# Loading q and k of an attention kernel already transposed, spreading them by transfers, and ranking clusters in PSUM

## Chip, cores and metric

One core of a Trainium2 chip runs the whole program. The metric is the device time of one execution in microseconds; the median of three runs of the kernel before is 873.62 us (873.53 to 875.32).

## What is computed

Three layers, one after the other, all in float32. The attention has 16 heads (2 batches of 8), 768 tokens and a head dimension of 64. Every query and every key is assigned to the nearest of 16 centroids of its head, and a query sees only keys of its own cluster:

```python
q_assign = argmax(einsum('bhsd,hcd->bhsc', q_n, c_n))   # k_assign alike
mask = q_assign[:, :, :, None] == k_assign[:, :, None, :]
scores = where(mask, q @ k^T / 8, -1e9)
attn = softmax(scores);  x = attn @ v          # -> [1536 tokens, 512]
h = x @ w_in;  g = P(h) / Q(|h|);  y = g @ w_out            # 512 -> 2048 -> 512
out = (silu(y @ w_gate) * (y @ w_val)) @ w_out2             # 512 -> 1536 -> 512
```

## The kernel before

Every float32 factor of a matmul is split into a high part, rounded to the fast matmul type, and a low part, the rest; products of the parts are added in PSUM. The five engines each run their own list of instructions, written out by hand and tied by semaphores. The attention is a software pipeline over `STEPS`: step i brings the scores of tile i (128 queries of a head against its 768 keys), six steps to a head, and the later stages of older tiles follow with fixed lags. The two layers behind it (`mlps`, `mlp1`, `hidden`, `first_result`, `second_result`) come after the last step, except for four units of the first one that run in the last steps.

In one step TensorE (PE) issues the four score matmuls of its tile (L854, L857), six transposes of the probabilities of tile i-5 (L877) and a third of the product with v (L892, L894). VectorE (DVE) takes the row maximum (L699), and the low parts of the transposed probabilities (L719, two halves); every third step it adds an epsilon to three row sums (L708) and inverts them (L711), and once in three steps it forms x (L728). ScalarE (ACT) takes the exponential of the tile before (L513), the high parts of the transposed probabilities (L534) and half of x (L544). GpSimd (POOL) scales three tiles by their inverses every third step (L404), splits x (L412, L414), v (L422, L425), and the first six units of the weights of the first layer (L432, L434; one in each of the steps 23, 35, 47, 59, 90 and 93).

`head_at(step, stage)` names the head whose preparation has this stage at this step: stage s of head h falls at step 6h-13+s. In the kernel before they are:

- stage -1: POOL splits q and k, 128 tokens in the partitions (L391, L394), into `qk_split`
- stages 1 to 3: PE transposes four blocks of it each (L915), ACT copies them from PSUM to `qkT` (L558, L561), whose upper partitions so hold the high parts and whose lower ones hold the low parts
- stages 4 and 5: PE multiplies with the centroids (L933); ACT copies the low products (L576), DVE adds them (L734) and takes the maximum (L738)
- stage 6: DVE marks the maximum (L742), weighs by rank (L748) and takes the first (L752)
- stage 7: DVE makes the one-hot codes (L689); stage 8: PE transposes them (L866), ACT copies them to `clusterT` (L522, L524)

SyncE (SP) issues every DMA, in one queue. Its loop over heads waits for `qkT` of head h and for the scores of head h-2, issues four copies of 192 KB into `k_hihi` and `qk_low` (L294), waits for `clusterT` of head h, issues six copies of it (L297), and then the loads of q and k of head h+2 (L256), of v (L263) and, for the first four heads, of weights (L268, L271). The scores of head h wait for all ten copies (`s_dup`). Weight units 4 and up are loaded behind the attention's buffers that they replace.

Of the kernel before, what the change touches and what calls it, by code (L numbers as in the profile page):

```python
# [21 lines left out]
def build_program(nc, q, k, v, centroids, w_in, w_out1, a, b, w_gate, w_val, w_out2, out):  # L22
    P = 128
    B, H, S, D = q.shape
# [127 lines left out]
    HID, RES = 0, 4  # L152

# [13 lines left out]
    s_qkhi, s_qklo = sem("s_qkhi"), sem("s_qklo")  # L167
    s_tr, s_trc = sem("s_tr"), sem("s_trc")
# [24 lines left out]
    FIRST_STEP = -PREP_LEAD - 1  # L193
# [8 lines left out]
    def prep_bank(h, stage):  # L202

        return stage - 1 if h == 0 else PREP

# [40 lines left out]
    with block:  # L246

        @block.sync
        def _(sp):
            def load_qk(h):  # L250
                i, src = h % 2, (h // H, h % H)
                if h >= 2:

                    sp.wait_ge(s_qklo, h - 1)
                for n, t in enumerate((q, k)):
                    sp.dma_start(qk_raw[i][:, n, :, :],  # L256
                                 t[src[0], src[1]].rearrange("(p t) d -> p t d", t=T)
                                 ).then_inc(s_qk_in[i], 16)
# [21 lines left out]
            sp.dma_start(b_raw, b[None, :].to_broadcast([P, 2])).then_inc(s_par_in, 16)  # L280
            for h in range(NH):
                i = h % 2

                sp.wait_ge(s_trc, 3 * (h + 1))
# [4 lines left out]
                kT = qkT[h % 3][:, T:2 * T, :].rearrange("p t n -> p (t n)")  # L289
                qT = qkT[h % 3][:, 0:T, :].rearrange("p t n -> p (t n)")  # L290
# [16 lines left out]
            for u in range(EARLY, NF1):  # L307
                if w1_end(u) <= PREP_END:

                    sp.wait_ge(s_tr, 3 * NH)  # L310
                    sp.wait_ge(s_ohT, NH)
                    sp.wait_ge(s_dup[(NH - 1) % 2], DUPS * ((NH + 1) // 2))
                elif w1_end(u) <= PROB_END:
                    sp.wait_ge(s_pT, 2 * NT)
                else:
                    sp.wait_ge(s_xlo, NG)
# [12 lines left out]
            rows = out.rearrange("(c p t) d -> c t p d", c=B, t=T)  # L329
            for bl in range(NB):  # L330
                for tt in range(TT):
# [3 lines left out]
                    sp.dma_start(rows[tile // T, tile % T],  # L335
# [4 lines left out]
        def _(pool):  # L340
# [43 lines left out]
            for step in STEPS:  # L384
                h = head_at(step, -1)
                if h is not None:

                    pool.wait_ge(s_qk_in[h % 2], 32 * (h // 2 + 1))
                    if h:
                        pool.wait_ge(s_tr, 3 * h)  # L390
                    did(g.tensor_scalar(qk_split[:, :, :, 0, :].bitcast(F32R), qk_raw[h % 2][:, :, :, :],  # L391
                                        1.0, 1.0, ALU.mult, ALU.mult), s_qkhi)
                    pool.wait_ge(s_qkhi, h + 1)
                    did(g.tensor_tensor(qk_split[:, :, :, 1, :].bitcast(F32R), qk_raw[h % 2][:, :, :, :],  # L394
                                        qk_split[:, :, :, 0, :], ALU.subtract), s_qklo)
                    if h < 2:
                        g.memset(qk_low[h][0:D, :, :].bitcast(F32), 0.0).then_inc(s_zero, 1)

                if (step - HALF) % HALF == 0 and 0 <= (step - HALF) // HALF < NG:
                    half = (step - HALF) // HALF  # L400
                    pool.wait_ge(s_inv, half + 1)
                    for n in range(HALF):
                        i = (half * HALF + n) % T
                        did(g.tensor_scalar(prob[i][:, :], prob[i][:, :], row_inv[:, i:i + 1], 1.0,  # L404
                                        ALU.mult, ALU.mult), s_norm)
                g1, third = pv_at(step)
                if third == HALF - 1:

                    pool.wait_ge(s_xsum, g1 + 1)
                    finish_last()  # L410
                    xh, xl, raw = x_of(x_hi, g1), x_of(x_lo, g1), x_of(x_raw, g1)
                    did(g.tensor_scalar(xh, raw, 1.0, 1.0, ALU.mult, ALU.mult), s_xhi)  # L412
                    pool.wait_ge(s_xhi, g1 + 1)
# [28 lines left out]
        def _(sc):  # L442
# [62 lines left out]
            for step in STEPS:  # L505
# [10 lines left out]
                h = head_at(step, 8)  # L516
# [29 lines left out]
                for stage in (1, 2, 3):  # L546
                    h = head_at(step, stage)
                    if h is None:
                        continue

                    sc.wait_ge(s_tr, 3 * h + stage)
                    if h >= 3 and stage == 1:
                        sc.wait_ge(s_score, T * (h - 2))
                    n = 4 * (stage - 1)
                    nq = min(max(T - n, 0), 4)
                    src = ps[:, prep_bank(h, stage), :].rearrange("p (k n) -> p k n", k=4)
                    if nq:
                        ins = s.activation(qkT[h % 3][:, n:n + nq, :], src[:, 0:nq, :], ACT.Copy,  # L558
                                           scale=QSCALE)
                    if nq < 4:  # L560
                        ins = s.activation(qkT[h % 3][:, n + nq:n + 4, :], src[:, nq:4, :], ACT.Copy)  # L561
                    ins.then_inc(s_trc, 1)
                if head_at(step, 3) == 0:
# [6 lines left out]
                h = head_at(step, 5)  # L570
# [14 lines left out]
        def _(ve):  # L585
# [97 lines left out]
            for step in STEPS:  # L683
                h = head_at(step, 7)
                if h is not None:
                    if h:
                        ve.wait_ge(s_ohT, h)
                    ve.wait_ge(s_first, h + 1)
                    v_.tensor_tensor(onehot[:, :, :], ranked[:, :, :],  # L689
# [11 lines left out]
                if (step - HALF) % HALF == 0 and 0 <= (step - HALF) // HALF < NG:  # L701
# [29 lines left out]
                h = head_at(step, 5)  # L731
                if h is not None:
                    ve.wait_ge(s_logit_lo, h + 1)
                    v_.tensor_tensor(logit[:, :, :], ps[:, PREP, 0:4 * T * C].rearrange(  # L734
                        "p (n two c) -> p n two c", two=2, c=C)[:, :, 0, :], logit_lo[:, :, :],
                        ALU.add).then_inc(s_logit_sum, 1)
                    ve.wait_ge(s_logit_sum, h + 1)
                    v_.tensor_reduce(top[:, :], logit[:, :, :], AX.X, ALU.max).then_inc(s_top, 1)  # L738
                h = head_at(step, 6)
                if h is not None:  # L740
                    ve.wait_ge(s_top, h + 1)
                    v_.tensor_tensor(is_top[:, :, :], logit[:, :, :],  # L742
                                     top[:, :].unsqueeze(2).to_broadcast([P, 2 * T, C]),
                                     ALU.is_equal).then_inc(s_istop, 1)
# [3 lines left out]
                    v_.tensor_tensor(ranked[:, :, :], is_top[:, :, :],  # L748
                                     ramp[:, :].unsqueeze(1).to_broadcast([P, 2 * T, C]), ALU.mult
                                     ).then_inc(s_ranked, 1)  # L750
                    ve.wait_ge(s_ranked, h + 1)
# [227 lines left out]
```

## Time and profile before

| what | value |
|---|---|
| median of three runs | 873.62 us |
| the profiled execution | 873.85 us |
| its span, first to last instruction | 872.1 us |
| busy over the span: PE, DVE, ACT, POOL | 825.4, 545.5, 446.5, 383.5 us |
| mean granted TensorE clock | 0.996 of full speed |
| DMA: packets, bytes | 44012, 45.39 MB |

The busy time of an engine is the union of its instructions; PE's matmuls overlap, and their ends are modelled. "L404" is line 404 of the kernel before. In the rows below, what stands in brackets or behind the bar is the idle time of the engine ahead of an instruction and who ended it.

### The profile page before, as it was taken

What the parts mean: (1) busy time and instruction counts of PE and PEld (TensorE: products, weight loads), DVE (VectorE), ACT (ScalarE), POOL (GpSimd) and SP (SyncE); (2) the same over time, 40 slices, a digit from 0 to 9 for tenths busy, and PEclk for the clock granted to TensorE, in tenths of its full rate; (3) what the DMA queues carried; (4) which work ended last, traced back from release to release, by engine and by line L of the source; (5) the groups of instructions that cost most, each with busy time, mean ns of one, the idle gap of its engine ahead of it and who ended that gap; (6) DMA issues with size and microseconds to landing.
All of it is one profiled execution on the core that took longest, in us unless ns stands there. A gap on an engine that the chain in (4) does not pass through costs nothing.

```text
span 872.1 us, 11981 instructions
## 1 busy us (share of the span) xinstructions
PE 825.4 (95%) x4210; PEld 705.2 (81%) x4210; DVE 545.5 (63%) x911; ACT 446.5 (51%) x876; POOL 383.5 (44%) x352
## 2 busy tenths in 40 slices
PE   4789898898999989999999999999999999999998
PEld 3688887888888778888888888878888888888886
DVE  4698998988999868777877787753221321231222
ACT  3488777787788778777877787720000100010001
POOL 4467877878676849851222156696000000000000
PEclk9999999999999999999999999999999999999999
DMA  3634242232423034000000023340000100010001
GB/s 96 159 99 114 78 105 69 75 95 68 106 71 82 30 101 141 0 1 1 1 1 0 1 73 110 108 145 1 1 0 1 49 1 0 1 49 1 0 1 49
DMA packets 44012, 45.39 MB, mean 52 GB/s; under 512 B 5040, under 2 KB 34736, under 8 KB 43952
## 3 DMA queue, kind: packets, MB, share of 16 engines
q1 hardware_dynamic: 43952, 44.62, 18.2%
q8 instruction: 34, 0.56, 0.3%
q14 instruction: 26, 0.21, 0.1%
HBM read 27.30 MB, written 3.15 MB: 35 GB/s over the span
## 4 chain that ended last, share of the span: by engine, by line
PE 78%; DVE 14%; POOL 3%; issue 2%; ACT 1%; DMA 0%; SPq 0%; DVEq 0%; POOLq 0%; ACTq 0%
PE ps L766 17%; PE ps L765 17%; PE ps L767 17%; DVE neg_max L699 4%; PE ps L877 4%; PE ps L837 4%; PE ps L838 4%; PE ps L839 4%; DVE probT_lo L719 3%; PE ps L892 2%; PE ps L894 2%; PE ps L933 2%; PE ps L854 2%; PE ps L915 2%; PE ps L857 2%
## 5 line engine op out<-in xcount | busy, mean ns | idle before, releaser
L765 PE MATMUL ps<-x_hi,w_hi 128*128 128x512 f32 x480 | 186.8, 389 | 0.0
L766 PE MATMUL ps<-x_lo,w_hi 128*128 128x512 f32 x480 | 186.8, 389 | 0.0
L767 PE MATMUL ps<-x_hi,w_lo 128*128 128x512 f32 x480 | 186.7, 389 | 0.0
L671 DVE TENSOR_TENSOR act<-act,ps 128x512 f32<-128x512 f32 x36 | 24.8, 688 | 209.9 <-PE ps L767 209.9
L502 ACT ACTIVATE act<-ps 128x512 f32<-128x512 f32 x36 | 21.5, 598 | 249.5 <-PE ps L767 249.5
L366 POOL TENSOR_TENSOR den<-den,mag 128x512 f32<-128x512 f32 x48 | 62.3, 1299 | 122.5 <-ACT den L463 122.2
L404 POOL TENSOR_SCALAR prob<-prob,row_inv 128x768 f32<-128x768 f32 x96 | 85.8, 911 | 49.7 <-DVE row_inv L711 49.6
L877 PE MATMUL ps<-ident,prob 128*128 128x128 f32 x576 | 82.5, 279 | 24.4 <-DVE probT_lo L719 22.6
L767 PEld LDWEIGHTS ps<-x_hi,w_lo 128*128 128x128 f32 x480 | 90.1, 188 | 18.8
L765 PEld LDWEIGHTS ps<-x_hi,w_hi 128*128 128x128 f32 x480 | 90.1, 188 | 18.7
L766 PEld LDWEIGHTS ps<-x_lo,w_hi 128*128 128x128 f32 x480 | 90.1, 188 | 18.5
L719 DVE TENSOR_TENSOR probT_lo<-ps,probT_hi 128x384 fp32r<-128x384 f32 x192 | 97.3, 548 | 11.5 <-ACT probT_hi L534 11.3
L699 DVE TENSOR_REDUCE neg_max<-ps 128x1 f32<-128x768 f32 x96 | 91.4, 952 | 16.2 <-PE ps L857 14.8
L534 ACT ACTIVATE probT_hi<-ps 128x384 fp32r<-128x384 f32 x192 | 84.5, 493 | 25.1 <-PE ps L877 23.2
L877 PEld LDWEIGHTS ps<-ident,prob 128*128 128x128 f32 x576 | 65.9, 141 | 38.0 <-issue 29.1
L513 ACT ACTIVATE prob<-ps,neg_max 128x768 f32<-128x768 f32 x96 | 86.9, 905 | 15.2 <-DVE neg_max L699 14.7
L765 PE MATMUL ps<-g_hi,w_hi 128*128 128x512 f32 x192 | 74.7, 389 | 0.0
L766 PE MATMUL ps<-g_lo,w_hi 128*128 128x512 f32 x192 | 74.7, 389 | 0.0
L767 PE MATMUL ps<-g_hi,w_lo 128*128 128x512 f32 x192 | 74.7, 389 | 0.0
L892 PE MATMUL ps<-probT_hi,v_split 128*128 128x384 f32 x192 | 73.2, 381 | 1.3 <-DVE x_raw L728 1.3
L894 PE MATMUL ps<-probT_lo,v_split 128*128 128x384 f32 x192 | 65.2, 339 | 0.0
L854 PE MATMUL ps<-k_hihi,qkT 128*128 128x384 f32 x192 | 57.4, 381 | 0.2
(98 smaller groups left out, 1555.6 us busy)
## 6 DMA issues: line engine op xcount, KB each, us to landing
w_raw<-in_moe_w_out SPq DMA_DIRECT2D x28, 256.0 KB, 4.2
k_hihi<-qkT SPq DMA_DIRECT2D x32, 192.0 KB, 3.0
qk_low<-qkT SPq DMA_DIRECT2D x32, 192.0 KB, 3.7
w_raw<-in_moe_w_in SPq DMA_DIRECT2D x16, 256.0 KB, 3.9
qk_raw<-in_q SPq DMA_DIRECT2D x16, 192.0 KB, 2.7
qk_raw<-in_k SPq DMA_DIRECT2D x16, 192.0 KB, 2.6
v_raw<-in_v SPq DMA_DIRECT2D x16, 192.0 KB, 3.2
w_raw<-in_moe_w_gate SPq DMA_DIRECT2D x12, 256.0 KB, 3.1
```

The source lines that it names most:

```text
L404: did(g.tensor_scalar(prob[i][:, :], prob[i][:, :], row_inv[:, i:i + 1], 1.0, ALU.mult, ALU.mult), s_norm)
L513: s.activation(prob[i % T][:, :].rearrange("p (c n) -> p c n", c=2), ps[:, bank:bank + 2, 0:HC], ACT.Exp, bias=neg_max[:, i % T:i % T + 1] ...
L534: s.activation(probT_hi[g % 2][:, n * HALF:(n + 1) * HALF, c:c + P], ps[:, PT_BANK + n, 0:HC].rearrange("p (k n) -> p k n", k=HALF), ACT.C ...
L699: v_.tensor_reduce(neg_max[:, i % T:i % T + 1], ps[:, bank:bank + 2, 0:HC], AX.XY, ALU.max, negate=True).then_inc(s_max, 1)
L719: v_.tensor_tensor(probT_lo[g % 2][:, keys, c:c + P], ps[:, PT_BANK + n, 0:HC].rearrange("p (k n) -> p k n", k=HALF), probT_hi[g % 2][:, k ...
L765: mm(dst, hi, m_hi, start=start, stop=False)
L766: mm(dst, hi, m_lo, start=False, stop=False)
L767: return mm(dst, lo, m_hi, start=False, stop=stop)
L854: mm(ps[:, bank + c, 0:HC], qkT[h % 3][:, t, :], k_hihi[sl][:, c * HC:(c + 1) * HC], start=True, stop=False)
L877: last = transpose(ps[:, PT_BANK + n, kt % HALF * P:(kt % HALF + 1) * P], prob[i % T][:, kt * P:(kt + 1) * P], ident[:, :])
L892: mm(ps[:, O_BANK, 0:HC], vv, probT_hi[g % 2][:, kt, :], start=(kt == 0), stop=False)
L894: last = mm(ps[:, O_BANK, 0:HC], vv, probT_lo[g % 2][:, kt, :], start=False, stop=(kt == T - 1))
```

## The change

q arrives in DRAM as [head, 64, 768], and k likewise with its tokens in the order that the transposed tiles had (the host lays them out before the launch, so no device time is in that). One load puts q into the upper 64 partitions of `qk_raw` and k into the lower ones. POOL scales q by 1/8 in place, ACT rounds both to `qk_hi`, POOL subtracts for `qk_lo`, and SP spreads the parts by four transfers of 192 KB per head into `qkT`. The 12 transposes and four ACT copies per head are gone. The sums and codes of the ranking stay in the PSUM bank that held the products, and the ranking is cut at other steps; the last copy of the codes comes one step later. The epsilon of the row sums moves from DVE to POOL. x is split once for two heads, 128 partitions at a time. `PREP_END` shrinks, so `POOL_UNITS` is 5 in place of 6: weight unit 5 is loaded and split behind the attention. q's tokens keep their natural order, so the rows of the output do, too. Stages in the changed kernel: scale and high part 0, low part 2, products 4 and 5, sum 6, rank 7, first and one-hot 8, cluster 9.

```diff
     place = region(W_AT + EARLY * 8 * U1, T_AT)
-    qk_raw = [place(f"qk_raw{i}", [P, 2, T, D]) for i in range(2)]
-    qk_split = place("qk_split", [P, 2, T, 2, D])
+    raw_at = [cursor[0] + i * 4 * S for i in range(2)]
+    qk_raw = [place(f"qk_raw{i}", [P, S]) for i in range(2)]
+    qk_lo = [at(f"qk_lo{i}", [P, S], F32R, raw_at[i]) for i in range(2)]
+    qk_hi = [place(f"qk_hi{i}", [P, S], F32R) for i in range(2)]
     logit_lo = place("logit_lo", [P, 2 * T, C])
-    logit = place("logit", [P, 2 * T, C])
-    is_top = place("is_top", [P, 2 * T, C])
-    ranked = place("ranked", [P, 2 * T, C])
...
+    pair = ps[:, PREP, 0:4 * T * C].rearrange("p (n two c) -> p n two c", two=2, c=C)
+    logit, is_top = pair[:, :, 0, :], pair[:, :, 1, :]
...
+    S_SCALE, S_HI, S_LO, S_CEN, S_LOGIT, S_SUM, S_RANK, S_FIRST, S_CLUSTER = 0, 0, 2, 3, 4, 6, 7, 8, 9
+    def qkT_ready(h):
+        return s_qkT_in[h % 3], 64 * (h // 3 + 1)
+    def x_pair(x, h):
+        col = (h // H) * S
+        return x[:, (h % H) // 2, col:col + S]
...
@@ SP @@
+                    sp.wait_ge(*qkT_ready(h - 2))
+                    sp.dma_start(qk_raw[i][n * D:(n + 1) * D, :], t[src[0], src[1]]
+            def spread_qk(h):
+                i, dst = h % 2, qkT[h % 3].rearrange("p t n -> p (t n)")
+                if h >= 3:
+                    sp.wait_ge(s_score, T * (h - 2))
+                sp.wait_ge(s_qkhi, h + 1)
+                for n in range(2):
+                    sp.dma_start(dst[0:D, n * S:(n + 1) * S].bitcast(F32),
+                                 qk_hi[i][n * D:(n + 1) * D, :].bitcast(F32)
+                                 ).then_inc(s_qkT_in[h % 3], 16)
+                sp.wait_ge(s_qklo, h + 1)
+                for n in range(2):
+                    sp.dma_start(dst[D:P, n * S:(n + 1) * S].bitcast(F32),
+                                 qk_lo[i][n * D:(n + 1) * D, :].bitcast(F32)
+                                 ).then_inc(s_qkT_in[h % 3], 16)
+            spread_qk(0)
             for h in range(NH):
-                sp.wait_ge(s_trc, 3 * (h + 1))
+                sp.wait_ge(*qkT_ready(h))
...
                     sp.dma_start(dst.bitcast(F32), src.bitcast(F32)).then_inc(s_dup[i], 16)
+                if h + 1 < NH:
+                    spread_qk(h + 1)
                 sp.wait_ge(s_cluster, 2 * (h + 1))
@@ POOL, ahead of the steps @@
+            for i in range(2):
+                g.memset(qk_low[i][0:D, :, :].bitcast(F32), 0.0).then_inc(s_zero, 1)
@@ POOL, in a step: scale of q; epsilon and scaling of prob; low part; x; v; weights @@
+                h = head_at(step, S_SCALE)
+                    pool.wait_ge(s_qk_in[h % 2], 32 * (h // 2 + 1))
+                    did(g.tensor_scalar(qk_raw[h % 2][0:D, :], qk_raw[h % 2][0:D, :], QSCALE, 1.0,
+                                        ALU.mult, ALU.mult), s_qscale)
...
+                    pool.wait_ge(s_exp, HALF * (half + 1))
+                    did(g.tensor_scalar(row_den[:, c:c + HALF], row_sum[:, c:c + HALF], EPS_SUM, 1.0,
+                                        ALU.add, ALU.mult), s_den)
                     pool.wait_ge(s_inv, half + 1)
...
+                h = head_at(step, S_LO)
+                    pool.wait_ge(s_qkhi, h + 1)
+                    did(g.tensor_tensor(qk_lo[h % 2][:, :], qk_raw[h % 2][:, :],
+                                        qk_hi[h % 2][:, :].bitcast(F32), ALU.subtract), s_qklo)
-                if third == HALF - 1:
+                if third == HALF - 1 and g1 % 4 == 3:
...
-                    xh, xl, raw = x_of(x_hi, g1), x_of(x_lo, g1), x_of(x_raw, g1)
+                    xh, xl, raw = x_pair(x_hi, h), x_pair(x_lo, h), x_pair(x_raw, h)
@@ ACT, in a step behind exp, cluster copies, high parts of prob and x_part; logit_lo (S_SUM) follows @@
+                h = head_at(step, S_HI)
+                    sc.wait_ge(s_qscale, h + 1)
+                    if h >= 2:
+                        sc.wait_ge(*qkT_ready(h - 2))
+                    s.activation(qk_hi[h % 2][:, :], qk_raw[h % 2][:, :], ACT.Copy).then_inc(s_qkhi, 1)
...
@@ DVE @@
-                    ve.wait_ge(s_exp, HALF * (half + 1))
-                    v_.tensor_scalar(row_den[:, c:c + HALF], row_sum[:, c:c + HALF], EPS_SUM, None,
-                                     ALU.add).then_inc(s_den, 1)
                     ve.wait_ge(s_den, half + 1)
+                    v_.tensor_tensor(logit, logit, logit_lo[:, :, :], ALU.add).then_inc(s_logit_sum, 1)
+                    v_.tensor_tensor(is_top, logit, top[:, :].unsqueeze(2).to_broadcast([P, 2 * T, C]),
+                    v_.tensor_tensor(is_top, is_top, ramp[:, :].unsqueeze(1).to_broadcast([P, 2 * T, C]),
@@ PE: stages 1 to 3 are gone; ahead of the products with the centroids @@
-                    pe.wait_ge(s_trc, 3 * h + 3)
+                    pe.wait_ge(*qkT_ready(h))
+                    if h:
+                        pe.wait_ge(s_cluster, 2 * h)
```

## Rows read from the trace of the kernel before

**Rows 1.** Windows between starts of L711; columns: stretch, length, busy by engine, PEclk, DMA share, GB/s.

```profile
61.12:256.93 195.81, 177.40 (x1210) 164.76 (x1210) 176.56 (x331) 153.71 (x364) 152.43 (x162) 0.98 0.33 87
223.06:239.90 16.84, 15.72 (x110) 14.71 (x110) 15.40 (x31) 13.95 (x34) 12.76 (x14) 1.00 0.35 89
78.16:96.57 18.41, 15.77 (x110) 14.73 (x110) 16.98 (x30) 15.18 (x37) 16.16 (x16) 1.00 0.31 82
256.93:273.06 16.13, 15.10 (x106) 14.38 (x106) 14.71 (x30) 13.34 (x33) 9.92 (x12) 1.00 0.27 67
```

**Rows 2.** Chain that ended last, one head: start us, us, what.

```profile
225.45 0.44 PE ps L915 x4
...
230.45 0.57 PE ps L933 x6
...
237.02 1.06 DVE ranked L748
...
238.84 0.95 DVE neg_max L699
```

**Rows 3.** Groups of DVE instructions by form, whole span; behind the bar busy us, mean ns.

```profile
L742 DVE TENSOR_TENSOR is_top<-logit,top 128x192 f32<-128x192 f32 x16 | 11.5, 718 | 0.1
L748 DVE TENSOR_TENSOR ranked<-is_top,ramp 128x192 f32<-128x192 f32 x16 | 11.4, 713 | 0.6
L708 DVE TENSOR_SCALAR row_den<-row_sum 128x3 f32<-128x3 f32 x32 | 11.0, 345 | 0.2 <-ACT prob L513 0.2
...
L734 DVE TENSOR_TENSOR logit<-ps,logit_lo 128x192 f32<-128x192 f32 x16 | 5.6, 350 | 10.1 <-ACT logit_lo L576 9.9
```

**Rows 4.** Timeline of POOL in the same head: start us, us, instruction.

```profile
223.42 2.68 POOL L404 TENSOR_SCALAR prob<-prob,row_inv 128x768 f32<-128x768 f32 x3 [2.79 <-DVE row_inv L711]
```

**Rows 5.** Groups of POOL instructions by form, whole span.

```profile
L394 POOL TENSOR_TENSOR qk_split<-qk_raw,qk_split 128x768 fp32r<-128x768 f32 x16 | 29.3, 1832 | 1.3
...
L434 POOL TENSOR_TENSOR w_lo<-w_raw,w_hi 128x1024 fp32r<-128x1024 f32 x6 | 14.2, 2360 | 0.5
L391 POOL TENSOR_SCALAR qk_split<-qk_raw 128x768 fp32r<-128x768 f32 x16 | 13.4, 837 | 15.1 <-DMA qk_raw<-in_k 13.3 <-PE ps L915 1.7
...
L432 POOL TENSOR_SCALAR w_hi<-w_raw 128x1024 fp32r<-128x1024 f32 x6 | 6.3, 1049 | 0.4
```

**Rows 6.** Timeline of SP in the same head: start us, us of issuing, what.

```profile
224.33 3.85 SPq L297 DMA_DIRECT2D qk_low<-clusterT  x6
...
228.85 0.43 SPq L256 DMA_DIRECT2D qk_raw<-in_k  x1
...
234.62 1.16 SPq L294 DMA_DIRECT2D k_hihi<-qkT  x2
```

**Rows 7.** Page, DMA issues: count, KB each, median us from issue to landing.

```profile
k_hihi<-qkT SPq DMA_DIRECT2D x32, 192.0 KB, 3.0
qk_low<-qkT SPq DMA_DIRECT2D x32, 192.0 KB, 3.7
...
qk_raw<-in_k SPq DMA_DIRECT2D x16, 192.0 KB, 2.6
```

**Rows 8.** Groups of ACT instructions by form, whole span.

```profile
L513 ACT ACTIVATE prob<-ps,neg_max 128x768 f32<-128x768 f32 x96 | 86.9, 905 | 15.2 <-DVE neg_max L699 14.7
...
L576 ACT ACTIVATE logit_lo<-ps 128x192 f32<-128x192 f32 x16 | 5.3, 332 | 7.3 <-PE ps L933 6.2
```

**Rows 9.** Timelines of ACT and PE at the start.

```profile
8.31 0.87 ACT L558 ACTIVATE qkT<-ps 128x512 fp32r<-128x512 f32 x2
...
10.88 2.71 PE L933 MATMUL ps<-cenT,qkT 128*128 128x32 f32 x12 [0.63 <-ACT cenT L567]
```

**Rows 10.** Windows in and behind a long wait of PE, columns as in rows 1.

```profile
130.00:132.00 2.00, 0.20 (x2) 0.00 (x0) 1.97 (x2) 1.32 (x4) 1.95 (x1) 1.00 0.00 0
...
134.00:136.00 2.00, 2.00 (x10) 1.91 (x9) 1.43 (x3) 1.13 (x4) 1.08 (x3) 0.50 0.12 29
```

**Rows 11.** Timeline of POOL at the start of the second layer.

```profile
327.90 1.29 POOL L366 TENSOR_TENSOR den<-den,mag 128x512 f32<-128x512 f32 x1 [2.83 <-ACT den L463]
```

More of the change, by code:

```diff
@@ L23, in build_program @@
     P = 128
-    B, H, S, D = q.shape
+    B, H, D, S = q.shape
     C = centroids.shape[1]
@@ L166, in build_program @@
     s_cen_a, s_cen_v, s_cen_t, s_cen = sem("s_cen_a"), sem("s_cen_v"), sem("s_cen_t"), sem("s_cen")
-    s_qkhi, s_qklo = sem("s_qkhi"), sem("s_qklo")
-    s_tr, s_trc = sem("s_tr"), sem("s_trc")
+    s_qscale, s_qkhi, s_qklo = sem("s_qscale"), sem("s_qkhi"), sem("s_qklo")
+    s_qkT_in = [sem(f"s_qkT_in{i}") for i in range(3)]
     s_logit, s_top, s_istop, s_ranked, s_first, s_onehot = (sem(x) for x in (
@@ L328, in _ @@
                 sp.dma_start(w2_raw[j][:, 2 * DM:U2], w_out2[cols, :]).then_inc(s_w2_in[j], 16)
[L329 removed]
+            rows = out.rearrange("(n p) d -> n p d", p=P)
             for bl in range(NB):
@@ L334, in _ @@
                     sp.wait_ge(s_ov if tt % 2 else s_oa, (bl * TT + tt) // 2 + 1)
-                    sp.dma_start(rows[tile // T, tile % T],
+                    sp.dma_start(rows[tile],
                                  out_rows[:, tt, bl * TB:(bl + 1) * TB]).then_inc(s_out, 16)
@@ L515, in _ @@
                                  accum_out=row_sum[:, i % T:i % T + 1]).then_inc(s_exp, 1)
-                h = head_at(step, 8)
+                h = head_at(step, S_CLUSTER)
                 if h is not None:
@@ L545, in _ @@
                                  ).then_inc(s_xpart, 1)
[L546 to L563, printed above, removed]
+                h = head_at(step, S_HI)
+                if h is not None:
+                    sc.wait_ge(s_qscale, h + 1)
+                    if h >= 2:
+                        sc.wait_ge(*qkT_ready(h - 2))
+                    s.activation(qk_hi[h % 2][:, :], qk_raw[h % 2][:, :], ACT.Copy).then_inc(s_qkhi, 1)
+                if head_at(step, S_CEN) == 0:
                     sc.wait_ge(s_cen_t, 2)
@@ L569, in _ @@
                                      ACT.Copy).then_inc(s_cen, 1)
-                h = head_at(step, 5)
+                h = head_at(step, S_SUM)
                 if h is not None:
@@ L683, in _ @@
             for step in STEPS:
-                h = head_at(step, 7)
+                h = head_at(step, S_FIRST)
                 if h is not None:
+                    ve.wait_ge(s_ranked, h + 1)
+                    v_.tensor_reduce(first[:, :], is_top, AX.X, ALU.max).then_inc(s_first, 1)
+                    ve.wait_ge(s_first, h + 1)
                     if h:
                         ve.wait_ge(s_ohT, h)
-                    ve.wait_ge(s_first, h + 1)
-                    v_.tensor_tensor(onehot[:, :, :], ranked[:, :, :],
+                    v_.tensor_tensor(onehot[:, :, :], is_top,
                                      first[:, :].unsqueeze(2).to_broadcast([P, 2 * T, C]),
@@ L747, in _ @@
                     ve.wait_ge(s_istop, h + 1)
[L748 to L751, printed above, removed]
-                    v_.tensor_reduce(first[:, :], ranked[:, :, :], AX.X, ALU.max
-                                     ).then_inc(s_first, 1)
+                    v_.tensor_tensor(is_top, is_top, ramp[:, :].unsqueeze(1).to_broadcast([P, 2 * T, C]),
+                                     ALU.mult).then_inc(s_ranked, 1)
                 if step in TAIL:
@@ L897, in _ @@
                         last.then_inc(s_pv, 1)
-                for stage in (1, 2, 3):
-                    h = head_at(step, stage)
-                    if h is None:
-                        continue
-                    if stage == 1:
-                        pe.wait_ge(s_qklo, h + 1)
-                        if h:
-                            pe.wait_ge(s_logit_sum, h)
-                        else:
-                            pe.wait_ge(s_const, C + 1)
-                    elif h:
-                        pe.wait_ge(s_trc, 3 * h + stage - 1)
-                        if stage == 2 and h:
-                            pe.wait_ge(s_cluster, 2 * h)
-                    for n in range(4):
-                        nn = 4 * (stage - 1) + n
-                        src = qk_split[:, nn // T, nn % T, :, :].rearrange("p a d -> p (a d)")
-                        last = transpose(ps[:, prep_bank(h, stage), n * P:(n + 1) * P], src,
-                                         ident[:, :])
-                    last.then_inc(s_tr, 1)
-                if head_at(step, 3) == 0:
+                if head_at(step, S_CEN) == 0:
+                    pe.wait_ge(s_const, C + 1)
                     pe.wait_ge(s_cen_v, 13)
@@ L968 @@
     for name in _INS:
-        x = _np.ascontiguousarray(inputs[name])
+        x = inputs[name]
+        if name == "q":
+            x = x.transpose(0, 1, 3, 2)
+        if name == "k":
+            x = x.reshape(*x.shape[:2], 128, -1, x.shape[3]).transpose(0, 1, 4, 3, 2).reshape(
+                *x.shape[:2], x.shape[3], -1)
+        x = _np.ascontiguousarray(x)
         arrays[f"in_{name}"] = x
```

53 lines of the change are left out of this document (19 added, 34 removed).

## Prediction

> **What bounds the kernel now.** I read the windows first, to see how even the attention is. Between the inverse at step 12 and the one at step 78 lie 11 heads and 195.8 us. A plain head takes 16.84 to 17.03 us, one with a weight split on POOL 18.41. In the plain head PE is busy 15.72 us and DVE 15.40, so both are nearly full, and neither is quite the bound [rows 1]. The two layers behind the attention are PE's own matmuls, and the change touches only their first weights.
>
> Then the chain of waits, over one head. It goes in two stretches of some 8 us: first along PE, with the transposes of `qk_split` in it twice (0.44 us each) and one set of products with the centroids (0.57), then along DVE, with `ranked` at 1.06 us and the row maximum behind the whole ranking [rows 2]. The groups say why `ranked` is long: it and `is_top` average 0.71 us, though the sum of the same 192 elements with an operand in PSUM takes 0.35; the epsilon averages 0.345 for three elements [rows 3]. These are the ones that meet a POOL instruction.
>
> **The change, part by part, as a saving.** PE loses 12 transposes a head, by the chain three times 0.44 = 1.3 us of work, of which 0.9 is on the chain [rows 2]. DVE loses 2 x 0.345 of epsilon and, with the ranking in PSUM, some 0.36 each of `is_top` and `ranked`: 1.4 us. Of the new PSUM forms no row exists; the sum at 0.35 is the nearest, and at worst they stay at 0.71, off the chain. The ranking also moves: on DVE it stood on the chain ahead of the inverse of step 0, from 237.02 to 238.84 with `is_top` (0.3) before it, 2.1 us [rows 2]; now rank and first code lie behind the inverse, where the chain runs along PE. If nothing else bound, a head would need what PE and DVE have to do, 15.72 - 1.3 and 15.40 - 1.4, so about 14.4 us, with the stalls of today 15.3. ACT trades four copies for one. x's splits shrink from two short pairs a head to one long pair in two heads; this costs nothing while POOL has the 2.79 us that it waits today for the inverse [rows 4]. The epsilon on POOL costs DVE nothing as long as POOL arrives before DVE; it does so by that same 2.79.
>
> **The change as a loop.** The new order makes a circle through POOL, SP, a load, POOL, ACT and DVE that is exactly one head long. I follow it from the start of an inverse at a step divisible by six.
>
> 1. POOL starts scaling `prob` 0.36 us after it (223.06 to 223.42) and takes 2.68 for three tiles [rows 1, 4]; then the low part of q and k, 1.83 [rows 5]. That is 4.87.
> 2. SP has stood at the wait for this low part. It issues its two spreads, 1.16 for a pair [rows 6]: 6.05. The cluster codes of the head before are there by then; but they were queued behind this wait.
> 3. From the first of six cluster copies to the issue of the load of k SP needs 4.52 (224.33 to 228.85) [rows 6]: 10.6.
> 4. The load lands. Loads of k take 2.6, but go to 128 partitions; transfers of the same size to 64 partitions, as the new load is, take 3.0, or 3.7 when queued [rows 7]. It shares its source with the first and its shape with the second, so I take 2.8: 13.4. Ends: 2.6 and 3.7.
> 5. POOL scales, 0.84 [rows 5]: 14.25. ACT, which has waited for that, rounds 768 columns. No row shows a copy of this width; an exponential of it takes 0.905 [rows 8], and as instructions overlap by 0.1 I take 0.8 until the next one starts (0.7 to 0.9): 15.05.
> 6. Behind it on ACT stands `logit_lo`, 0.33 [rows 8], for which DVE waits: the sum and the maximum of the ranking, 0.35 each [rows 3], then the row maximum of the tile, 0.95 [rows 2]: 17.0. Then the next inverse.
>
> So the loop gives 17.0 us a head against 17.03 now. What PE and DVE save is waited away: PE and DVE will be less busy, ACT will wait for the scale, POOL for the load.
>
> In four heads the weight split (1.05 + 2.36 and gaps, 3.5) [rows 5] stands on POOL between the scale and the epsilon. From 14.25 that gives 17.75, with 0.2 for the epsilon (it was 0.345 on DVE; the ends are nothing and that) 18.0, against 18.41.
>
> A second loop runs over the products: the last spread is issued at 5.5 and lands at 8.5 (3.0) or 9.2 (3.7) [rows 6, 7]. From the first products at 230.45 to the next inverse at 239.90 are 9.45 us now [rows 1, 2]; without the 2.1 us of ranking 7.35. That makes 15.9 to 16.6: below the first, but not by much.
>
> The Trainium skill's page "SBUF — State Buffer" (Door 1: The DMA port swizzle) says that a transfer to 64 partitions reaches only half of the 16 ports. The gap between 3.0 and 2.6 in rows 7 fits that. By its 435 GB/s for all ports, 192 KB would take 0.9 us in place of 0.45, so the load 3.05; taken whole, this rule would add about 0.25 us to each loop, 3 us in all.
>
> **The sum.** Eleven heads: seven by 17.0 and four by 18.0 are 191.0, so 4.8 less. Two of the four heads with a split were followed by a stretch at the lower clock: PE stood for 1.8 of 2 us, and soon ran at 0.50 of full speed, 1.2 GHz [rows 10]; I count that as gone within the 4.8, since the wait there gets shorter. At the start ACT's first copy is at 8.31, held by a table load [rows 9], and the high part can't be earlier. Then 0.8, the low part 1.83, a spread 0.6 and 2.8 to 3.0: products at about 14.4, where they were at 10.88 [rows 9]. Of these 3.5 us some hides, since the first scores waited for more than this; ends are 0 and 3.5 plus a late load, I take +2.5. The last head with preparation (16.13) [rows 1] has no load behind it, and the second loop gives 15.9 to 16.6: nothing. At the end one weight split fewer delays POOL, -0.5. Unit 5, now loaded and split at the start of the second layer, costs POOL 3.5 us more there, beside 2.83 of idle [rows 11] and a stretch in which PE has work of its own; nothing, or up to 2 us if that cover is gone. Sum: -4.8 + 2.5 - 0.5 = -2.8. The profiled execution took 873.85, 0.2 above the median; so 871.0.
>
> About 0.2% (1.75 us) is what a measurement of this kernel can tell from no change.
>
> **Rivals.**
>
> *The circle isn't closed* (chance 0.26). If loads land early enough or DVE finishes ahead of the loop, PE and DVE set the pace at 15.3 us. For it: both are near full now, and the ranking leaves the chain. Against it: every term of the loop is a duration of this trace. Seven heads by 15.3 and four by 16.7 are 174, 22 less; with the start and end 853.
>
> *The loop is longer, and the kernel slower* (0.22). Its place is SP: behind the wait for the low part stand the six cluster copies and then the load, whose landing everything waits for. It decides from a landing of 3.0 us on, since 2.8 us over some 13 loops are 0.2 each. At the 3.7 that queued copies show [rows 7] each of 13 loops is 0.9 longer: 882.5. For it: four more transfers a head in the same queue, and 64 partitions.
>
> *The clock* (0.04). With 14.4 us to do in 17.0, PE waits 2.6 us in each head. If that is one stretch like that of rows 10, the lower clock follows it and costs about 1.6 us each time: 889.
>
> That the change doesn't do what it says in one part, the ranking in PSUM still meeting POOL, would move neither: it has left the chain.
>
> **How the numbers follow.** My case has 0.48, its own range 866 to 877. Within it faster takes 0.24, same 0.14, slower 0.10. With the rivals that is faster 0.50, same 0.14, slower 0.36. The range of 8 in 10 reaches to 854 and 886, cutting half of the first rival's low side and the clock.
>
> **What would show it.** Right: windows between inverses of 17 us with PE and DVE each a good 1 us less busy; POOL's scale waiting for the DMA of k in nearly each head; the high part on ACT waiting for the scale, and DVE's sum for `logit_lo`; no epsilon or rank instruction on DVE above 0.5 us; the first products near 14.4 us. Wrong: heads of 15.5 us or less and no wait for a load; PE's waits ended by the spread, which would make the second loop the bound; a landing far from 2.8; or a second layer that waits for its weights.

## The result, and the profile after

The changed kernel takes 885.9 us (median of 4 runs, 884.46 to 886.6), the kernel before beside it 874.42 (873.53 to 875.32): a ratio of 1.0129, interval 1.011 to 1.0148. So it is 1.3% slower, where 0.3% faster was forecast; the range of 854 to 886 holds it at its edge. One execution of a kernel below, the one with the low part at step 0, took 1624 us and is in no ratio.

The windows of the changed kernel, from one inverse to the next (columns as in [rows 1]): the 11 heads, a plain head, a head with an x pair in it (x split for two heads at once), the last head with preparation, and the steps 90 to 96.

```profile
65.12:265.34 200.22, 169.94 (x1080) 149.22 (x1079) 158.82 (x310) 144.26 (x331) 135.76 (x150) 0.99 0.52 130
137.80:155.85 18.05, 14.90 (x98) 13.48 (x98) 14.37 (x29) 12.06 (x28) 9.87 (x12) 1.00 0.51 130
229.67:247.19 17.52, 15.53 (x100) 13.30 (x99) 14.44 (x29) 13.16 (x31) 12.57 (x14) 1.00 0.47 115
265.34:282.31 16.97, 14.98 (x97) 12.93 (x97) 14.35 (x30) 12.50 (x30) 11.74 (x13) 1.00 0.35 84
296.27:311.78 15.51, 13.26 (x83) 11.47 (x82) 11.66 (x23) 11.92 (x27) 13.36 (x14) 1.00 0.00 1
```

The 11 heads take 200.22 us where they took 195.81 [rows 1]; DVE is busy 14.4 us in a plain head, 1 us less than before, and PE 14.9, 0.8 less. The work left the engines as planned, and the head got longer. By the inverses (45.00, 61.12, 256.93 and 300.26 before at steps 6, 12, 78 and 96; 47.59, 65.12, 265.34 and 311.78 now): +4.0 up to step 12, +4.4 in the 11 heads, +3.1 from step 78 to 96. Behind that lie 571.8 us of the span before and 570.8 now, -1.0. Together the 10.5 by which the span grew, 872.1 to 882.6.

The waits of the changed kernel from 60 to 330 us say what the heads wait for (engine, instruction, releaser: us in total, times, longest).

```profile
POOL qk_raw L410 <- DMA qk_raw<-in_k: 33.9, 12, 4.2
POOL row_den L419 <- ACT prob L538: 27.7, 17, 3.2
...
DVE row_inv L724 <- POOL row_den L419: 19.9, 12, 2.0
...
DVE ps L747 <- ACT logit_lo L590: 13.3, 12, 1.8
...
ACT qk_hi L576 <- POOL qk_raw L410: 9.4, 8, 1.5
...
PEld ps L922 <- DMA qkT<-qk_lo: 7.1, 12, 1.0
```

POOL waits for the load of k once in each head: the circle of the prediction is closed. Two lines lie outside it. DVE waits 12 times for the epsilon on POOL: seven times 2.0 us behind an x pair, four times 1.1 behind a weight split, and once 1.5 at the end. And PE waits for the spread.

The chain of waits over one head, one with a weight split, from inverse to inverse:

```profile
155.85 0.18 DVE row_inv L724
156.02 0.09 issue
156.11 2.68 POOL prob L424 x3
158.79 1.79 POOL qk_lo L429
160.59 0.02 issue
160.60 0.46 SPq L274
...
166.29 0.59 SPq L260
166.88 0.04 issue
166.93 3.81 DMA qk_raw<-in_k
170.74 0.08 issue
170.82 0.83 POOL qk_raw L410
171.65 1.02 POOL w_hi L457
...
172.75 2.37 POOL w_lo L459
175.12 0.08 issue
175.20 0.21 POOL row_den L419
...
175.50 0.18 DVE row_inv L724
```

It is the loop in the order in which the prediction wrote it, in its longest head (19.65 us). What differs most is the landing: 3.81 us, not 2.8. The table of DMA issues of the changed kernel gives the medians (KB, then us to landing; before in [rows 7]):

```profile
qkT<-qk_lo SPq DMA_DIRECT2D x32, 192.0 KB, 3.0
...
qk_raw<-in_q SPq DMA_DIRECT2D x16, 192.0 KB, 3.3
qk_raw<-in_k SPq DMA_DIRECT2D x16, 192.0 KB, 3.5
```

The loads of k went from 2.6 to 3.5. On DVE the ranking no longer meets POOL (by groups; before in [rows 3], 718 and 713 ns):

```profile
L758 DVE TENSOR_TENSOR ps<-ps,ramp 128x192 f32<-128x192 f32 x16 | 5.9, 367 | 0.6
L753 DVE TENSOR_TENSOR ps<-ps,top 128x192 f32<-128x192 f32 x16 | 5.7, 356 | 0.0
```

And the place where the epsilon hurts, in the timelines of POOL and DVE in the head from 155.85:

```profile
161.78 1.83 POOL L439 TENSOR_TENSOR x_lo<-x_raw,x_hi 128x768 fp32r<-128x768 f32 x1
163.70 0.51 POOL L447 TENSOR_SCALAR v_split<-v_raw 128x384 fp32r<-128x384 f32 x1
164.30 1.00 POOL L450 TENSOR_TENSOR v_split<-v_raw,v_split 128x384 fp32r<-128x384 f32 x1
165.38 0.20 POOL L419 TENSOR_SCALAR row_den<-row_sum 128x3 f32<-128x3 f32 x1
```
```profile
165.68 0.18 DVE L724 RECIPROCAL row_inv<-row_den 128x3 f32<-128x3 f32 x1 [2.01 <-POOL row_den L419]
```

POOL has no gap above 0.1 us there: the x pair and the split of v fill it, and an instruction of 0.20 us holds DVE for 2.01.

### The profile page after: what moved, and what is told of

Its sections match the earlier page's. It is cut to its first block, busy times and chain, and to the rows that moved or that the text cites. A ratio compares the mean times of both kernels' runs of the same rounds, so it can differ in the third digit from the quotient of the medians.

```text
span 882.6 us, 11538 instructions
## 1 busy us (share of the span) xinstructions
PE 813.0 (92%) x4018; PEld 684.7 (78%) x4018; DVE 519.5 (59%) x879; ACT 432.7 (49%) x828; POOL 361.1 (41%) x336
## 4 chain that ended last, share of the span: by engine, by line
PE 69%; POOL 10%; DVE 6%; issue 5%; DMA 4%; SPq 3%; ACT 1%; ACTq 0%; POOLq 0%; DVEq 0%
PE ps L771 17%; PE ps L772 17%; PE ps L773 17%; POOL prob L424 4%; PE ps L843 4%; PE ps L844 4%; PE ps L845 4%; SPq L318 2%; PE ps L883 2%; DMA qk_raw<-in_k 2%; DMA qkT<-qk_lo 2%; POOL qk_lo L429 2%; DVE probT_lo L732 2%; DVE neg_max L715 1%; POOL w_lo L459 1%
## 5 line engine op out<-in xcount | busy, mean ns | idle before, releaser
L883 PE MATMUL ps<-ident,prob 128*128 128x128 f32 x576 | 84.8, 283 | 27.1 <-DVE probT_lo L732 27.1
```

The lines of the kernel that those rows point to most:

```text
L883: last = transpose(ps[:, PT_BANK + n, kt % HALF * P:(kt % HALF + 1) * P], prob[i % T][:, kt * P:(kt + 1) * P], ident[:, :])
```

## The experiments

The theory after the result: the loop sets the heads, with a landing that the 64 partitions lengthen (A). Its rivals: the landing is long from traffic, not from its form (B); the epsilon on POOL sets the time (C); something in the ranking or the x pair does (D). Each time below is a median, its ratio and interval are to the kernel before on the same chip (875.04 to 875.65 us there).

**Opening the circle.** `load_qk(h + 2)` goes from behind the cluster copies to the wait for the spread of head h:

```
                 sp.wait_ge(*qkT_ready(h))
+                if h + 2 < NH:
+                    load_qk(h + 2)
...
-                if h + 2 < NH:
-                    load_qk(h + 2)
```

> The changed kernel with one move in SP's queue: the loads of q and k of head h+2 are issued as soon as the spread of head h has landed, ahead of its four copies, in place of behind the spread of head h+1 and the six cluster copies. Theory (the circle through SP and the load sets the head): the wait of POOL for the DMA of k goes, the second loop over the spread and the products and, in every second head, the wait for the epsilon behind the split of x take over; plain heads fall from 17.5 to about 16 us, heads with a weight split from 18.5 to about 17.4, in all some 15 us less than the changed kernel, 868 to 872 us. Rival 1 (the epsilon on POOL is the cause): the wait for it stays and so does the time, 884 to 886. Rival 2 (more DMA traffic slows everything): little moves, 883 or more.

Measured: 870.27 us, 0.9947 (0.9929 to 0.9966). The 11 heads, window of that kernel:

```profile
63.81:250.27 186.46, 166.67 (x1080) 147.87 (x1079) 158.76 (x309) 143.18 (x331) 135.13 (x150) 1.00 0.55 137
```

13.8 us less in 11 heads, with the landing of k as long as before (median 3.6): POOL no longer waits for it there. So the loop set the heads. By the inverses, the six heads without an x pair now take 16.4 to 16.7 us, the five with one 17.3 to 17.5. PE waits for the spread 12 times, 8.0 us: the second loop is next.

**A shorter way behind the scale.** On ACT `logit_lo`, for which DVE waits, goes ahead of the rounding `qk_hi`:

```
-                    s.activation(qk_hi[h % 2][:, :], qk_raw[h % 2][:, :], ACT.Copy).then_inc(s_qkhi, 1)
...
                         ).then_inc(s_logit_lo, 1)
+                h = head_at(step, S_HI)
+                ...
+                    s.activation(qk_hi[h % 2][:, :], qk_raw[h % 2][:, :], ACT.Copy).then_inc(s_qkhi, 1)
```

> The changed kernel with ACT's copy of the low products issued ahead of the rounding of q and k in the same step. Theory: it leaves the circle a shorter closing, over the exponential and the epsilon on POOL in place of the ranking on DVE; by the rows 0.3 to 0.7 us a head, 4 to 8 us in all, 878 to 882. Rival (epsilon or traffic): no change, within 1 us of 885.9.

Measured: 880.33, 1.0063 (1.0039 to 1.0087), 5.6 us less. So what stands between the scale and the ranking lies on the loop too, as steps 5 and 6 have it: from the scale to the next inverse a plain head takes 2.97 us in place of 3.50, in the mean of seven.

**Form or traffic?** The kernel before, with its loads in the new form:

```
-                    sp.dma_start(qk_raw[i][:, n, :, :],
-                                 t[src[0], src[1]].rearrange("(p t) d -> p t d", t=T)
+                    sp.dma_start(qk_raw[i][n * D:(n + 1) * D, :, :, :].rearrange("p n t d -> p (n t d)"),
+                                 t[src[0], src[1]].rearrange("(p t) d -> p (t d)", t=2 * T)
```

> The kernel before, with q and k each loaded as 64 rows of 3072 bytes to 64 partitions, as the changed kernel does, so that what it computes from them is of tokens in the wrong places; nothing else differs. If the form makes the load slow, its landing rises from 2.6 to about 3.3 to 3.5 us and its issue from 0.43 to 0.6; if the traffic of the changed kernel does, it stays at 2.6. Time about the same as before either way, up to 3 us more since POOL had little spare time ahead of its split.

One run of 878.19 us, where the kernel before took 875.4. The DMA issues of that kernel:

```profile
qk_raw<-in_q SPq DMA_DIRECT2D x16, 192.0 KB, 3.3
qk_raw<-in_k SPq DMA_DIRECT2D x16, 192.0 KB, 3.5
```

The same as in the changed kernel, without its other transfers. Then the reverse, the changed kernel with its loads to 128 partitions:

```
-                    sp.dma_start(qk_raw[i][n * D:(n + 1) * D, :], t[src[0], src[1]]
+                    sp.dma_start(qk_raw[i][:, n * S // 2:(n + 1) * S // 2],
+                                 t[src[0], src[1]].rearrange("d (a s) -> (d a) s", a=2)
```

> The changed kernel, with q and k each loaded to all 128 partitions (half of the columns), so that its ranking and scores are of wrong numbers; queue, order and bytes stay. Theory (the circle through SP and the load, with a landing of 3.5 where 2.6 was to be had): landing falls back to about 2.6 and the issue of k to 0.43, so each head gets 1 us shorter until the second loop at 16.5 takes over; 9 to 13 us less than the changed kernel, 873 to 877. Rival (traffic of the added transfers): landing and time stay, 884 to 886.

```profile
qk_raw<-in_q SPq DMA_DIRECT2D x16, 192.0 KB, 2.6
qk_raw<-in_k SPq DMA_DIRECT2D x16, 192.0 KB, 2.5
```

Measured: 874.7, 0.9995 (0.9983 to 1.0006): 11.2 us less than the changed kernel, by the form of 32 loads alone. Its 11 heads:

```profile
64.19:254.91 190.72, 167.71 (x1079) 147.80 (x1079) 158.78 (x309) 143.59 (x331) 135.46 (x150) 1.00 0.54 136
```

POOL still waits for the load in each of them, so the loop still sets them, with a shorter landing. A holds, B falls. One thing stays open in A: the new form has half the partitions and rows twice as long (64 of 3072 bytes for 128 of 1536), and no run separates the two.

**The epsilon.** In the changed kernel back on DVE:

```
-                    did(g.tensor_scalar(row_den[:, c:c + HALF], row_sum[:, c:c + HALF], EPS_SUM, 1.0,
-                                        ALU.add, ALU.mult), s_den)
+                    v_.tensor_scalar(row_den[:, c:c + HALF], row_sum[:, c:c + HALF], EPS_SUM, None,
+                                     ALU.add).then_inc(s_den, 1)
```

> The changed kernel with the epsilon of the row sums back on DVE, the rest as changed. Theory (circle through the load): the wait of DVE for the epsilon behind the split of x (2.0 us, seven times) goes, but the heads keep their length, since the circle does not pass it; 0 to 4 us less, 882 to 886. Rival 1 (the epsilon on POOL is the cause): 10 us or more less, 876 or below.

Measured: 884.26, 1.0115 (1.0088 to 1.0142), 1.6 us less, and the intervals overlap, so this is not told from nothing. The heads keep their length, 199.95 us for the 11 (66.00 to 265.95) against 200.22. C falls as the cause of the longer heads: the wait of 2.0 us stands in a loop that would wait anyway.

**The parts alone, in the kernel before.** First the ranking in PSUM:

```
-                    v_.tensor_tensor(ranked[:, :, :], is_top[:, :, :],
+                    v_.tensor_tensor(p_top, p_top,
...
-                            pe.wait_ge(s_logit_sum, h)
+                            pe.wait_ge(s_onehot, h)
```

> The kernel before with one part of the change alone: the ranking kept in the PSUM bank of the products, at the old steps; PE's transposes of the next head then wait for the one-hot codes in place of the sum. Theory: is_top and ranked fall from 0.71 to 0.36 us, on the chain; less what PE waits for the bank, some 0.3 us a head; 3 to 8 us less than the kernel before, 867 to 872. Rival (the wait for the bank eats it): no change or up to 5 us more.

Measured: 865.38, 0.9898 (0.9875 to 0.9922), 10 us less than before and more than expected. This is the part that earns. To it are added the epsilon on POOL, the x pair, and both:

> The kernel before with the ranking in PSUM, and the epsilon of the row sums on POOL besides. If the epsilon on DVE costs by meeting the long weight splits of POOL (1.46 us in four heads), it makes little difference, since on POOL it stands behind the same split: 0 to 3 us less than the ranking alone (865.4), 862 to 866. If the hand-over itself costs, up to 3 us more.

Measured: 875.36, 0.9997 (0.9986 to 1.0008). A miss: 10 us more than the ranking alone, where 3 less to 3 more was expected. The waits of that kernel, 60 to 330 us, and POOL's timeline at the end of the attention:

```profile
DVE row_inv L716 <- POOL row_den L407: 22.0, 19, 3.6
```
```profile
287.54 1.05 POOL L440 TENSOR_SCALAR w_hi<-w_raw 128x1024 fp32r<-128x1024 f32 x1
288.67 2.39 POOL L442 TENSOR_TENSOR w_lo<-w_raw,w_hi 128x1024 fp32r<-128x1024 f32 x1
291.23 0.51 POOL L420 TENSOR_SCALAR x_hi<-x_raw 64x384 fp32r<-64x384 f32 x1 [0.17 <-POOL w_lo L442]
291.82 1.00 POOL L422 TENSOR_TENSOR x_lo<-x_raw,x_hi 64x384 fp32r<-64x384 f32 x1
292.91 0.51 POOL L430 TENSOR_SCALAR v_split<-v_raw 128x384 fp32r<-128x384 f32 x1
293.51 0.99 POOL L433 TENSOR_TENSOR v_split<-v_raw,v_split 128x384 fp32r<-128x384 f32 x1
294.58 0.20 POOL L407 TENSOR_SCALAR row_den<-row_sum 128x3 f32<-128x3 f32 x1
```

Seven microseconds of splits stand ahead of 0.20 us, for which DVE waits 3.60.

> The kernel before with the ranking in PSUM, and x split once for two heads besides, the epsilon on DVE. In the heads with a weight split POOL loses 1.5 us of work ahead of the epsilon; these heads are 18.2 us against 16.35 of the others, and I expect them at about 16.7: 4 to 7 us less than the ranking alone, 858 to 862. Rival (POOL was never what made them long): no change.

Measured: 859.72, 0.9822 (0.9807 to 0.9837), with the epsilon on DVE. The x pair brings 5.7 us, as expected, and this is faster than both kernels of the case. The trace says where: in the four heads with a weight split the epsilon on DVE meets that split on POOL and takes 2.2 us with the ranking alone and 1.1 with the x pair, against 0.16 in most of the others. So the epsilon costs something on either engine. The 11 heads:

```profile
60.21:243.01 182.80, 174.84 (x1212) 161.05 (x1212) 167.03 (x330) 151.17 (x364) 131.17 (x128) 1.00 0.36 93
```

> All parts of the change but the load and the spread: ranking in PSUM, epsilon on POOL, x split once for two heads. Theory (only the load and spread made the change slow): about 10 us or more less than the kernel before, near the better of the two others, 856 to 862. Rival (the epsilon behind the long split of x costs 2 us in every second head here too): 866 or more.

Measured: 868.26, 0.9921 (0.9906 to 0.9935): the epsilon on POOL costs 8.5 us beside the x pair. With the one before, D falls: both parts help in the kernel before. The new steps of the ranking were not tried alone.

**With the load early, what is left?** Two kernels with the early load and the epsilon on DVE, the second with the low part at step 0 of a head in place of step 2:

```
-    S_SCALE, S_HI, S_LO, S_CEN, S_LOGIT, S_SUM, S_RANK, S_FIRST, S_CLUSTER = 0, 0, 2, 3, 4, 6, 7, 8, 9
+    S_SCALE, S_HI, S_LO, S_CEN, S_LOGIT, S_SUM, S_RANK, S_FIRST, S_CLUSTER = 0, 0, 0, 3, 4, 6, 7, 8, 9
```

> The changed kernel with both mends: the load ahead of the copies, and the epsilon back on DVE. Theory (two causes, the circle first, and behind it the epsilon, which the circle hid): the waits of DVE for the epsilon (eight times 2 us in the version with the early load) go, and the end of the attention gets some 3 us shorter; 5 to 9 us less than the early load alone (870.3), 861 to 865. Rival (the second loop over the spread and the products is what is left): 868 or more, heads at 16.5 all the same.

Measured: 866.5, 0.9898 (0.9881 to 0.9916), 3.8 less than with the epsilon on POOL, just above what was expected. PE still waits for the spread:

```profile
PEld ps L920 <- DMA qkT<-qk_lo: 6.7, 11, 1.0
```

> The same, with the low part on POOL at the step of the scale and the high part, ahead of the scaling of the probabilities in place of behind it. If the second loop (low part, spread, products) sets the head in the version with both mends, PE's wait for the DMA of the low part goes and a head loses up to 0.7 us, 3 to 8 us in all. Against it: POOL then waits for ACT's rounding, and the low part stands ahead of the scaling; if that weighs more, the time is the same or up to 8 us more, with PE's transposes waiting for POOL's scaled probabilities.

Measured: 861.15, 0.9818 (0.979 to 0.9846). The wait for the spread is gone and 11 heads take 178.73 us, 16.25 each. The kernel without this move takes 183.70 for them. So the second loop was real, and was the bound once the first was open.

**Two that failed.** The early load, with the x pair split two steps later and the early weight splits six steps earlier:

```
-    pool_split_at = {u: 2 * T * (u + 2) - 1 for u in range(EARLY)}
+    pool_split_at = {u: 2 * T * (u + 2) - 7 for u in range(EARLY)}
...
-                g1, third = pv_at(step)
+                g1, third = pv_at(step - 2)
```

> The early load, and on POOL the split of x for two heads two steps later and the four early weight splits six steps earlier, so that each falls between the scaling at a step 3 and the epsilon at a step 0 in different heads. Theory (the long split ahead of the epsilon costs DVE 2 us in every second head, which makes that head 17.5 in place of 16.5): nearly all of that goes, 4 to 6 us less than the early load alone, 864 to 867 us. Rival (the heads with a split are long because the spread lands late, as in the others): no change, 869 to 871.

Measured: 870.4, 0.9954 (0.9939 to 0.9969), nothing gained. DVE's wait for the epsilon was gone inside the heads and came back as one of 4.2 us at their end, the heads stayed at 16.4 to 17.5 us, and PE waited for the spread 8.2 us in 11 places. The second loop stood behind the first, and the low part's own step had not been moved yet.

On top of that the scale and the high part one step earlier and the low part at step 0, then the same with the epsilon on DVE:

```
-    FIRST_STEP = -PREP_LEAD
+    FIRST_STEP = -PREP_LEAD - 1
...
-    S_SCALE, S_HI, S_LO, S_CEN, S_LOGIT, S_SUM, S_RANK, S_FIRST, S_CLUSTER = 0, 0, 2, 3, 4, 6, 7, 8, 9
+    S_SCALE, S_HI, S_LO, S_CEN, S_LOGIT, S_SUM, S_RANK, S_FIRST, S_CLUSTER = -1, -1, 0, 3, 4, 6, 7, 8, 9
```

> The same, and the scale and the high part one step earlier and the low part two steps earlier, so that the spread has landed long before the products need it. Theory (with the load early, the second loop over low part, spread and products sets plain heads at 16.5): the wait of PE for the DMA of the low part goes, and heads fall to what PE and DVE have to do with the stalls of the kernel before, 15 to 15.6 us; 12 to 20 us less than the version before it, 846 to 853 us. Rival 1 (PE and DVE are the bound at 16.5 already): within 2 us of the version before it, 862 to 867. Rival 2 (POOL becomes the bound, since two parts now stand ahead of the epsilon): heads of 16 us with DVE waiting for the epsilon in each, 858 to 862.

> The version with the low part early, and the epsilon of the row sums back on DVE. Theory: with the circles gone, what the move of the epsilon is worth shows: on POOL it waits for the exponential and for POOL's own work, on DVE it meets POOL's long instructions; I expect 1 to 4 us less if DVE waits for POOL's epsilon in most heads of the other version, 1 to 4 us more if it waits in few.

Measured: 882.62, 1.0093 (1.0067 to 1.0118), and 881.49, 1.0083 (1.0062 to 1.0104). The first missed its 846 to 853 by 30 us; the second differs from it by 1.1 us, which is not clear of noise. The windows of two heads of the first of them, and a wait from 60 to 330 us:

```profile
155.34:174.63 19.29, 14.86 (x91) 13.44 (x92) 14.44 (x29) 11.76 (x27) 12.54 (x14) 0.93 0.55 131
174.63:192.53 17.90, 16.42 (x106) 15.05 (x105) 14.37 (x30) 14.13 (x33) 13.28 (x14) 0.98 0.45 107
```
```profile
ACT qk_hi L576 <- POOL qk_raw L410: 15.1, 5, 3.0
```

One step earlier POOL's scale stands behind the scaling of `prob` (2.69) and the x pair (0.83 + 1.85), and ACT waits for it, up to 3.0 us, with the exponentials of the next tiles queued behind. The load was early; the queues weren't. The granted clock of the first window is 0.93, so part of its length may be the clock's; no run separates this. The kernel with the low part at step 0 alone, above, shows that this part isn't what costs; that the earlier scale alone is, was not run by itself.

## Why the prediction was wrong, step by step

**The loop was right, and one term was mis-sized.** Mean of the 11 heads of the changed kernel, from the timelines of SP, POOL and DVE:

| step of the prediction | predicted | measured |
|---|---|---|
| 1, 2, 3: inverse to the issue of k's load | 10.6 | 10.64 (10.45 to 11.09) |
| 4: landing, to the start of the scale | 2.8 | 3.63 (3.29 to 4.09) |
| 5, 6: scale to the next inverse, plain head | 3.6 | 3.50 |
| the same, head with a weight split | 4.6 | 4.70 |
| plain head (7) / split head (4) | 17.0 / 18.0 | 17.86 / 18.81 |
| 11 heads | 191.0 | 200.2 |

The failed step is number 4, "it shares its source with the first and its shape with the second, so I take 2.8". The form of the new load decides alone: 3.5 with the traffic of either kernel. 11 times 0.83 is 9.1 of the 9.2 us by which the heads were missed. Of the whole miss, 13.3 us (-2.8 forecast, +10.5 in the span), the heads are 9.2, the start 1.5, the end 3.6 and the second layer -1.0. With a landing of 2.5 the 11 heads take 190.72, my 191.0, partly by luck: my landing was 2.8, and by my own sum 2.5 would have given less. That kernel came out even with the kernel before (874.7) and above my 871.0, by the terms below. Both ends, 2.6 and 3.7, stood in the prediction with rows, and the nearer row was the one with 64 partitions.

The Trainium skill's rule (page "SBUF — State Buffer", Door 1: The DMA port swizzle), that 64 partitions reach half of the ports, was the warning. The runs agree with its direction, and the effect was larger than the 0.45 us that I had estimated from it: 0.7 for q (2.6 and 3.3 in the changed kernel with either form) and 1.0 for k (2.5 and 3.5). As the length of the rows changed with the partitions, they do not show that the ports are the whole cause.

**The start, +2.5 predicted, +4.0 measured at step 12.** The first products came at 13.70 (forecast 14.4), and the inverse of step 6 is 2.6 later than before (47.59 against 45.00), the predicted figure. The other 1.4 come in the head from step 6 to 12, 17.53 us against 16.12: it is the twelfth turn of the loop, and it was not in my sum, which began the loop at step 12.

**The last head with preparation, "nothing", and the end, -0.5.** Measured +3.1 from step 78 to 96. The last head takes 16.97, above the 15.9 to 16.6 of the second loop (+0.84 to before); DVE waits 2.02 us for the epsilon in it. From step 90 to 93 it is 8.68 us against 6.60: POOL's x pair and v split stand ahead of the epsilon there, and DVE waits 2.02 us.

**"The epsilon on POOL costs DVE nothing as long as POOL arrives before DVE."** The condition was right and the reading of it wrong. The 2.79 us of [rows 4] are from one head; with the x pair, whose 2.67 us I let lie in the same 2.79, POOL arrives last seven times. (The four times behind a weight split were in my sum.) Two edits were paid from one cover. Inside the closed circle the price is not told from nothing (1.6 us), with the load early it is 3.8, and in the kernel before with the ranking in PSUM 8.5 to 10.

**The x pair, "costs nothing".** It brings 5.7 us where the circle isn't there. **The ranking, 1.4 us of DVE a head:** measured 0.356 and 0.367 us, as taken. "It has left the chain" held for the loop, but in the kernel before it is on the chain, and 10 us come of it. I had these gains in hand (15.3 us a head if nothing else bound) and gave them to the loop; rightly so: the kernel before with the ranking in PSUM at its old steps and the x pair takes 859.72, 26.2 us less than the whole change.

**The second layer's weights, "nothing, or up to 2 us":** behind step 96 the changed kernel is 1.0 us shorter.

**The rivals.** "The loop is longer, and the kernel slower" was right in its place and nearly in its price, 882.5 against 885.9; the chance of 0.22 was too low. It put the point from which it decides at a landing of 3.0 us, but with 2.5 the kernel is already only even, since the start and the end cost more than I had for them. The first rival's 853 is 854 by its own terms. Its pace, heads at 15.3, is not reached by any kernel here: the best have 16.25 and 16.6. The lower clock: the changed kernel's granted clock in the heads is 0.99, and it isn't what made it slower.

**Left open:** whether the partitions or the length of the rows make the load slow, what holds the heads of the two best versions at 16.3 to 16.6 us, and what of the 30 us of miss lies in the earlier scale alone. The early load was not tried with a form that lands in 2.5 us.

## What to carry to other kernels

When a change makes a loop of latencies exactly one period long, its period is the sum of the terms, and work taken off the busy engines is worth nothing until the loop is open; issue the load ahead of the waits of the same period and it is gone (15.6 us here for a move of two lines). Of two rows that share one property each with a new transfer, plan with the slower one, and count every turn of the loop, those at the start and the end too. A tiny instruction moved to an engine that works through its queue in order costs what stands ahead of it, not its own time, and a gap of an engine can cover one edit only.

## What the hardware showed that I had not expected

- A load of 192 KB from HBM lands in 2.5 to 2.7 us as 128 rows to 128 partitions and in 3.2 to 3.6 as 64 rows to 64 (medians), in both kernels. SP needs 0.60 us to issue the load of k in the second form and 0.43 in the first [rows 6]; for q, issued just before it, 0.58 to 0.59 in either.
- The 0.71 us of `is_top` and `ranked` [rows 3] are a mean of two kinds. Some take 0.35 us. The others run into a subtraction on POOL and last until about 0.2 us after it is over, 1.05 us mostly and 1.86 at the longest. With the result and one operand in PSUM, at the same steps, none of the 32 takes more than 0.37, though the same subtraction runs beside them. First the kernel before, then the one with the ranking in PSUM:

```profile
219.63 1.00 POOL L414 TENSOR_TENSOR x_lo<-x_raw,x_hi 64x384 fp32r<-64x384 f32 x1
219.80 1.04 DVE L742 TENSOR_TENSOR is_top<-logit,top 128x192 f32<-128x192 f32 x1
```
```profile
109.52 1.00 POOL L416 TENSOR_TENSOR x_lo<-x_raw,x_hi 64x384 fp32r<-64x384 f32 x1
109.70 0.35 DVE L743 TENSOR_TENSOR ps<-ps,top 128x192 f32<-128x192 f32 x1
```
